# Identity multiplies in TensorE's waits ahead of the first unit's attention, in a fused attention and two-expert kernel

## The reference, cut to what matters

```
def _attn_ref(q, k, v, f_logit):
    f = 1.0 / (1.0 + np.exp(-f_logit))
    for t in range(S):
        state = f[:, :, t, :, None] * state + np.einsum('bhd,bhe->bhde', k[:, :, t], v[:, :, t])
        y[:, :, t] = np.einsum('bhd,bhde->bhe', q[:, :, t], state)

def _moe_ref(x, w_in, w_out):
    h = x @ w_in
    g = np.where(h >= 1, h, np.where(h <= -1, 0.0, (h + 1) ** 2 / 4))
    return g @ w_out

def _moe2_ref(x, w1, w2, w3, w_out):
    return ((x @ w1) * (x @ w2)) @ w3 @ w_out
```

## Time and profile before

| | us |
|---|---|
| median of 3 runs | 956.05 |
| lowest and highest | 955.44, 956.9 |
| the profiled execution's own time | 955.9 |
| its span, from the first to the last instruction | 954.0 |
| TensorE busy | 909.0 (95%) |
| mean granted TensorE clock | 0.983 of full speed |

### The profile page before, as it was taken

The page is one execution under the profiler, slowest core; times in us unless marked ns, Lnnn a source line. Parts: engine busy times, 40 slices in busy tenths (PEclk is TensorE's granted clock), DMA queues, the critical chain, the costliest instruction groups (busy, mean ns, idle before and its releaser), DMA issues.

```text
span 954.0 us, 23987 instructions
## 1 busy us (share of the span) xinstructions
PE 909.0 (95%) x10536; PEld 844.5 (89%) x10536; DVE 527.3 (55%) x956; ACT 392.8 (41%) x766; POOL 148.2 (16%) x151
## 2 busy tenths in 40 slices
PE   0679799999999999999999999999999999999998
PEld 0669699999999999999999999998888888888887
DVE  6655688866867767767767764464212221312222
ACT  1323365555544644645544544574222222222212
POOL 2320403403403404305205100000000000000000
PEclk9969899999999999999999999999999999999999
DMA  9930570160160250250340200512010102000000
GB/s 269 238 110 34 171 106 3 26 127 2 27 126 2 51 102 2 61 92 2 80 73 2 52 3 1 190 68 92 1 67 1 66 1 67 1 34 1 34 1 33
DMA packets 115831, 57.64 MB, mean 60 GB/s; under 512 B 92432, under 2 KB 111120, under 8 KB 115216
## 3 DMA queue, kind: packets, MB, share of 16 engines
q1 hardware_dynamic: 115728, 56.11, 24.6%
HBM read 45.09 MB, written 11.01 MB: 59 GB/s over the span
## 4 chain that ended last, share of the span: by engine, by line
PE 92%; DVE 5%; DMA 1%; issue 1%; ACT 1%; SPq 0%; DVEq 0%; ACTq 0%
PE bank L1076 17%; PE bank L1078 15%; PE bank L1077 15%; PE bank L1314 10%; PE bank L1313 10%; PE bank L1312 10%; PE bank L1014 4%; PE bank L1025 2%; PE bank L1051 2%; PE bank L1057 1%; PE bank L1038 1%; PE bank L983 1%; PE bank L988 1%; DMA first_q<-in_q_dram 1%; PE bank L993 1%; PE bank L1071 1%
## 5 line engine op out<-in xcount | busy, mean ns | idle before, releaser
L1282 DVE TENSOR_TENSOR product<-bank,a_copy 128x512 f32<-128x512 f32 x48 | 33.2, 692 | 221.1 <-PE bank L1314 221.1
L1076 PE MATMUL bank<-x_hi,w_in_hi 128*128 128x384 f32 x384 | 135.5, 353 | 0.5 <-DVE x_lo L897 0.5
L1076 PE MATMUL bank<-g_hi,w_out_hi 128*128 128x384 f32 x384 | 133.7, 348 | 0.3 <-DVE g_lo L908 0.3
L1078 PE MATMUL bank<-x_hi,w_in_lo 128*128 128x384 f32 x384 | 129.2, 337 | 0.0
L1077 PE MATMUL bank<-x_lo,w_in_hi 128*128 128x384 f32 x384 | 129.1, 336 | 0.0
L1078 PE MATMUL bank<-g_hi,w_out_lo 128*128 128x384 f32 x384 | 128.8, 335 | 0.0
L1077 PE MATMUL bank<-g_lo,w_out_hi 128*128 128x384 f32 x384 | 128.6, 335 | 0.0
L654 ACT ACTIVATE g_hi<-gated 128x384 fp32r<-128x384 f32 x128 | 67.2, 525 | 128.2 <-DVE gated L903 128.1
L1314 PE MATMUL bank<-y_hi,w_lo 128*128 128x512 f32 x288 | 112.8, 392 | 0.0
L1313 PE MATMUL bank<-y_lo,w_hi 128*128 128x512 f32 x288 | 112.7, 391 | 0.0
L1312 PE MATMUL bank<-y_hi,w_hi 128*128 128x512 f32 x288 | 112.0, 389 | 0.0
(11 more groups left out here) (113 smaller groups left out, 1697.5 us busy)
## 6 DMA issues: line engine op xcount, KB each, us to landing
v_leaf<-in_v_dram SPq DMA_DIRECT2D x8, 576.0 KB, 6.3
v_rows<-in_v_dram SPq DMA_DIRECT2D x64, 72.0 KB, 2.7
middle<-middle_out SPq DMA_DIRECT2D x8, 576.0 KB, 3.3
w_rows<-in_moe_w_dram SPq DMA_DIRECT2D x8, 512.0 KB, 10.4
f_leaf<-in_f_logit_dram SPq DMA_DIRECT2D x28, 144.0 KB, 3.9
k_leaf<-in_k_dram SPq DMA_DIRECT2D x28, 144.0 KB, 4.6
q_leaf<-in_q_dram SPq DMA_DIRECT2D x28, 144.0 KB, 4.4
out_dram<-out_rows SPq DMA_DIRECT2D x5, 768.0 KB, 4.0
```

The costliest lines, as they stand in the source:

```text
L1076: nc.tensor.matmul(o, w[0], b[0], start=first, stop=False)
L1078: return nc.tensor.matmul(o, w[1], b[0], start=False, stop=last_)
```

## The change

A helper `keep_running(n)` issues n multiplies of the identity (128x128, plain float32) by itself into `y_acc[2][:, 0:P]`, with start and stop set, and no semaphore. Nobody reads the result. It is called in five places, each time ahead of a wait: 40 multiplies ahead of turn 0, 12 ahead of turn 1, 12 ahead of the first join part, 9 ahead of level 1 and 20 ahead of level 3 of unit 0, 93 in all. Nothing else is changed, and no other engine has another instruction or another order.

```
+BEFORE_TURN, BEFORE_JOIN, BEFORE_LEVEL = {0: 40, 1: 12}, 12, (0, 9, 0, 20)
...
             def attention(grp, u):
                 kind, n = grp[0], grp[-1]
                 bank = bank_of(u, grp)
+                if u == 0 and kind == "level":
+                    keep_running(BEFORE_LEVEL[n])
                 wait_bank(pe, u, grp)
...
             def turn(t):
 
+                keep_running(BEFORE_TURN.get(t, 0))
                 pe.wait_ge(w3_in[t % 4], 16 * (t // 4 + 1))
...
                 if t == 0:
+                    if part == 0:
+                        keep_running(BEFORE_JOIN)
                     pe.wait_ge(wl_lo, T2 // 2 * (part + 1) // JOIN_PARTS)
...
+            def keep_running(n):
+
+                for _ in range(n):
+                    nc.tensor.matmul(y_acc[2][:, 0:P], ident[:], ident[:], start=True, stop=True)
```

## The result

| | before | changed |
|---|---|---|
| median, lowest and highest of 5 runs, us | 955.44 (954.28 to 956.9) | 949.93 (947.69 to 950.46) |
| ratio, 95% interval | | 0.9937 (0.9921 to 0.9952) |
| profiled execution, its span | 955.9, 954.0 | 947.69, 945.8 |
| mean granted clock of that execution | 0.983 | 0.991 |

The change makes the kernel 0.6% faster. The profiled execution of the changed kernel is the shortest of its five. The other four report mean clocks of 0.986 to 0.989 and times of 948.33 to 950.46.

What follows compares the result with a forecast made beforehand. TensorE bounds the kernel, busy 909.0 of 954.0 us, with gains possible only before 120 us. 0.9 + 1.7 + 1.5 + 4.45 = 8.55 off 955.9 gives 947.35, as a median 947.5; range 946.0 to 952.7.

Steps and rivals of the forecast that it cites:

- The price of a multiply: One identity multiply on TensorE: two records, taken as 0.215 us at the full clock and 0.43 at the half clock.
- They fit in the waits: All five fillings were to end inside their waits at cost 0, with 0 to 1 us allowed ahead of the first join.
- Step 1, turn 1 at full clock: Turn 1's eight transposes were to take 0.80 us instead of 1.73, moving the first join by 0.9 us.
- Step 2: The first twelve joins were to take 2.28 us instead of 4.00, a gain of 1.7 us.
- Step 3: Level 1 to the end of its join part: 3.02 us instead of 4.53, gain 1.5.
- Step 4: Level 3 to turn 4 at the full clock: 8.35 us instead of 12.80, gain 4.45.
- The sum: If the clock holds, the four gains total 8.55 us, taking the profiled execution from 955.9 to 947.35.
- the 1 us either way of the prediction: Behind the last join: allowance for the clock's last fall landing elsewhere in the work.
- the favoured case: The clock held to the end of the joins: 947.5 us, own range 946.0 to 949.0, chance 0.47.
- the first rival: Clock falls around level 3 or later, in the rest of the wait ahead of it: 949 to 952.7 us, chance 0.38.
- The slower rival: Multiplying an almost empty matrix doesn't raise the clock, so all fillings run slow: about 957.0 to 962 us, chance 0.05.
- fail to do what it says: The clock stays as it was in all places, since the waits' rests bring it down: 956 us, chance 0.07.

Runs made afterwards that it cites:

- first trace beside its parts: The changed kernel unaltered, measured again on another chip together with kernels that do part of its filling: 948.27 us, ratio 0.992 to the kernel before.
- the fully filled one: 44, 18, 16, 12 and 28 multiplies in place of the changed kernel's 40, 12, 12, 9 and 20: 948.66 us, ratio 0.9936 to the kernel before.
- the last kernel: Only the 9 and 20 multiplies ahead of levels 1 and 3, plus 16 ahead of turn 0: 950.36 us, ratio 0.9953 to the kernel before.

## Why the prediction came out as it did

- **The price of a multiply** held: two records, 0.22 us at the full clock, where 0.215 was taken. 40 of them took until 13.68 us (predicted near 13.6).
- **They fit in the waits** in all five places of the profiled execution. Ahead of the first join they don't where the clock is down when they start: in the changed kernel's first trace beside its parts VectorE's low parts began at 28.43, which would have released the join at 29.43, and it came at 29.91 without idle time ahead of it, 0.5 late. The prediction had allowed 0 to 1 there and taken 0. The kernel with 40 ahead of level 3 shows that too many are on the path.
- **Step 1, turn 1 at full clock**, was mis-sized. In the shortest execution the distance to the transposes of f was 1.00 us (1.73 before), so it gave 0.73 and not 0.9; the second half waits for VectorE's low parts. In five of the ten other traces that have the filling at the start (both of the changed kernel, the fully filled one, both with the waits behind the joins filled) the clock fell between 22 and 25 us and part or all of it was lost. The prediction took the wait ahead of turn 1 as harmless once filled at its front, and 1.9 to 3.7 us of its end stayed idle with twelve multiplies. The multiplies ahead of the join brought the clock back, as said, so step 2 was safe.
- **Step 2, the first twelve joins**: 31.07 - 28.85 = 2.22 us (2.28 predicted). They began at 28.85, 0.45 sooner than said: VectorE's q times f took 2.00 us and not the 2.50 of the earlier trace rows. It takes 2.50 to 2.58 in the three traces without filling ahead of turn 1 and 1.74 to 2.28 in the eleven with it; why is open. The transposes of k and q behind these joins also ran slow before, 36.63 - 34.22 = 2.41 us against 33.23 - 31.07 = 2.16, which the sum left out.
- **Step 3**: level 1 to the end of its join part took 47.00 - 44.01 = 2.99 (3.02 predicted).
- **Step 4**: 8.49 (8.35 predicted), with the 0.9 us wait ahead of krow. This was the largest term, and the run without the 20 multiplies shows it to be the clock's.
- **The sum** for an execution whose clock holds was 947.35, and the profiled execution took 947.69. Up to the update behind the joins it won 105.41 - 96.10 = 9.3 us and not 8.55 (0.45 from the earlier join, 0.25 from the transposes of k and q), then lost 1.1 again, where the clock was down for 13 us instead of 10 (the 1 us either way of the prediction). That the two ends lie 0.3 apart is in part luck: the two misses have opposite signs.
- **The slow start** was read rightly as 1.2 GHz, but from the lengths alone. No row of the kernel before has a granted clock of 0.50 there; the last kernel's trace shows it (12 to 36 us).
- **The forecast 947.5 was 2.4 us below the median 949.93.** The measured median lies in the stated range, but outside the favoured case's own (946.0 to 949.0) and in the one given to the first rival. It was the sum for one execution, and the median is of executions that differ. The first rival named that, but not how it went. A fall straight out of the rest of the wait ahead of level 3 that lasts to turn 4 was in none of the traces with that wait filled. What was there are short falls: near 22 us (1.1 us at the first join), and one during or behind level 3 for 3 to 7 us, in three of the eleven traces with that wait filled (0.3 to 2.1 us). On the two later chips the changed kernel's medians were 948.27 and 948.39. What made three of the first five runs take 949.93 to 950.46 is open: none of them was profiled, and the clock alone doesn't tell, since 948.33 and 950.45 report the same mean of 0.989. A standstill at level 2 is one candidate. The kernels with the waits behind the joins filled have the changed kernel's program up to there and stood still for 1.18 and 0.68 us.
- **The slower rival** (an almost empty matrix does not raise the clock) fell: the first 80 records of the identity took 10.83 us, where 0.216 us each, the half clock's length, would have made 17.3. Its price had left out turn 0: at 0.5 us each, 40 multiplies would have ended at 22.8 and turn 0 behind them at 24.8, 2 us after VectorE reads it. Neither did the change fail to do what it says.
- The kernel before was no fixed base either. Its 24 runs on one chip span 5 us, and they part by the clock: the seven that report 0.986 took 953.34 to 954.76, the ten that report 0.982 took 956.74 to 958.32. Its single profiled execution hid that. How long the clock stays down once it has fallen in the wait ahead of level 3 is one term that can differ: 17 us in that execution, 14 in the run without the 20 multiplies.

## What to carry to other kernels

Where a serial chain leaves a dense engine waiting, compare the start-to-start time of the same instruction in different stretches: work at half the clock shows as busy time, not as idle, and it lasts far beyond the wait that caused it. Fill such waits with harmless work whose length is known, nearly to their end, and leave a margin, since one multiply too many is on the path. Where the granted clock has not fallen yet in a trace, go by the length of the same work and not by the reading. Look at several executions before and after, because with a clock that falls by chance a single profile gives the best case or the worst, and the spread between runs is itself a sign of it.

## What the runs showed of the hardware

- With plain float32 operands of 128x128 a multiply is two records and takes 0.22 us at the full clock. A transpose is one record.
- Transposes alone bring the clock up and hold it (from 0.55 at 18 to 20 us to 1.00 at 20 to 28 us in the run with transposes).
- Ahead of the first fall in a trace the granted clock read 1.00 for work at either speed: 0.32 us per join at 32 to 34 us of the kernel before, and 0.50 for the same work in the last kernel.
- TensorE was busy 2.00 of 2.00 us in most stretches from 64 to 74 us of the kernel before, at half the clock throughout. From 62.93 to 75.7 it ran level 3, joins and krow one after another, and the granted clock came back only at 74 to 76.
- TensorE stood still without any wait of the program for 0.7 to 2.0 us in 5 of the 12 experiments' traces, most often seven records into level 2. These places, and a sixth of 0.18 us, lie multiples of 256 of TensorE's instructions apart. On the path a standstill costs its full length (level 2 was 2.2 us longer with the one of 2.00); in a filled wait the one of 1.56 us still cost 1.1, because the clock fell and the filling ended late.
